# Attention and dense layers on one core: transposes alternated with products of 64 stationary columns, the activation's sums in PSUM, the last products tile by tile

## What is computed

```python
# attention: 2 batches x 8 heads, 768 rows, 64 columns; 16 clusters
q_assign = argmax(q_n . c_n); k_assign = argmax(k_n . c_n)
scores = where(q_assign == k_assign, q @ k.T / 8, -1e9)
attn = softmax(scores) @ v
# sparse layer: 1536 rows x 512, 8 experts of 1024, best expert alone
out[mask] = gate_w * eom * (relu(x[mask] @ w1[e]) @ w2[e])
# dense layers: 512 -> 2048 -> 512
h = x @ w_in
g = where(h >= 1, h, where(h <= -1, 0, (h + 1) ** 2 / 4))
return g @ w_out
```

## Time and profile before

| | us |
|---|---|
| median of three runs | 934.82 |
| lowest and highest | 929.96, 935.59 |
| the profiled execution | 934.28 |
| its span in the trace | 932.5 |
| PE busy | 826.5 (89% of the span) |
| DVE busy | 536.7 (58%) |
| ACT busy | 379.3 (41%) |
| POOL busy | 326.0 (35%) |

### The profile page before, as it was taken

The page is one execution under the profiler, slowest core; times in us unless marked ns, Lnnn a source line. Parts: engine busy times, 40 slices in busy tenths (PEclk is TensorE's granted clock), DMA queues, the critical chain, the costliest instruction groups (busy, mean ns, idle before and its releaser), DMA issues.

```text
span 932.5 us, 13746 instructions
## 1 busy us (share of the span) xinstructions
PE 826.5 (89%) x4331; PEld 682.4 (73%) x4332; DVE 536.7 (58%) x863; ACT 379.3 (41%) x762; POOL 326.0 (35%) x346
## 2 busy tenths in 40 slices
PE   4799999999999950998997997996999999999995
PEld 3688788887888840777786786784788888888884
DVE  5688788888788873334454453335645545454442
ACT  3677788777887730221211211121222322232222
POOL 4233444334432016557863863767100010010001
PEclk8899999999999985999999998999999999999998
DMA  8000223000120034889985984968000010000001
GB/s 277 26 27 26 79 88 115 25 26 25 51 98 0 1 103 159 237 279 319 332 286 172 332 281 156 332 244 271 4 1 0 1 46 1 1 23 23 1 1 45
DMA packets 46388, 105.23 MB, mean 113 GB/s; under 512 B 6544, under 2 KB 12688, under 8 KB 45328
## 3 DMA queue, kind: packets, MB, share of 16 engines
q1 hardware_dynamic: 24656, 51.48, 16.0%
q0 software_dynamic: 17408, 48.26, 15.4%
q10 hardware_dynamic: 4288, 5.03, 2.0%
HBM read 98.45 MB, written 6.32 MB: 112 GB/s over the span
## 4 chain that ended last, share of the span: by engine, by line
PE 71%; DVE 12%; issue 5%; DMA 4%; ACT 4%; POOL 2%; DVEq 1%; ACTq 0%
PE ps L1359 14%; PE ps L1346 14%; PE ps L1306 9%; PE ps L1286 9%; PE ps L1136 5%; DMA x_in<-sorted_rows 4%; DVE coef L982 3%; PE ps L1092 3%; PE ps L1122 3%; PE ps L1152 3%; PE ps L1164 2%; PE ps L1123 2%; PE ps L1150 2%; PE ps L1079 2%; POOL sorted_rows L455 1%
## 5 line engine op out<-in xcount | busy, mean ns | idle before, releaser
L344 POOL TENSOR_TENSOR weights<-staging,weights 128x2048 fp32r<-128x2048 f32 x34 | 156.5, 4616 | 32.0 <-DMA weights<-in_moe_w 24.5
L1359 PE MATMUL ps<-weights,g_t 128*128 128x512 f32 x576 | 144.6, 400 | 9.0 <-DVE g_t L1053 9.0
L1346 PE MATMUL ps<-y_t,weights 128*128 128x512 f32 x576 | 141.5, 395 | 0.0
L1359 PEld LDWEIGHTS ps<-weights,g_t 128*128 128x128 f32 x576 | 108.6, 190 | 35.6 <-DVE g_t L1053 9.9
L1346 PEld LDWEIGHTS ps<-y_t,weights 128*128 128x128 f32 x576 | 108.2, 188 | 25.7
L1306 PE MATMUL ps<-weights,h_t 128*128 x456 | 114.1, 408 | 3.9 <-issue 3.8
L1286 PE MATMUL ps<-weights,x_t 128*128 x456 | 110.9, 400 | 2.0 <-DVE x_t L976 2.0
L850 DVE TENSOR_TENSOR p_t<-ps,p_t 128x384 fp32r<-128x384 f32 x192 | 100.0, 549 | 14.8 <-ACT p_t L563 13.6
L1306 PEld LDWEIGHTS ps<-weights,h_t 128*128 128x128 f32 x456 | 87.7, 196 | 24.5 <-issue 6.0
L499 POOL DMA_INDIRECT out<-y_sb,token_u x12 | 11.9, 994 | 256.1 <-ACT y_sb L695 254.0
L1286 PEld LDWEIGHTS ps<-weights,x_t 128*128 128x128 f32 x456 | 85.4, 191 | 20.4 <-issue 2.6
(11 more groups left out here) (148 smaller groups left out, 1143.1 us busy)
## 6 DMA issues: line engine op xcount, KB each, us to landing
weights<-in_moe_w POOLq DMA_DIRECT2D x32, 1024.0 KB, 8.2
staging<-in_moe_w SPq DMA_DIRECT2D x32, 1024.0 KB, 6.1
x_in<-sorted_rows ACTq DMA_DIRECT2D x19, 258.0 KB, 4.9
weights<-in_moe_w_in POOLq DMA_DIRECT2D x4, 1024.0 KB, 8.1
staging<-in_moe_w_in SPq DMA_DIRECT2D x4, 1024.0 KB, 5.8
staging<-in_moe_w_out SPq DMA_DIRECT2D x4, 1024.0 KB, 5.7
weights<-in_moe_w_out POOLq DMA_DIRECT2D x4, 1024.0 KB, 7.1
raw<-in_q SPq DMA_DIRECT2D x16, 192.0 KB, 2.6
```

The costliest lines, as they stand in the source:

```text
L344: pool.tensor_tensor(weights[:, unit % 2, 1, c * CHUNK:(c + 1) * CHUNK], staging[:, n % 2, :], hi.bitcast(F32), ALU.subtract).then_inc(w_r ...
L1346: last = mm(ps[:, 4 + n % 2, :], wi[:, a, k, f * P:(f + 1) * P], y_ts[g % 2][:, b, k, :], start=(k == 0 and j == 0), stop=(k == KC - 1 and ...
L1359: last = mm(ps[:, t, :], g_t[:, n % 2, a, t * P:(t + 1) * P], wo[:, b, f, :], start=(f == 0 and j == 0), stop=(f == FC2 - 1 and j == 2))
```

## The change

In attention PE's list is put in another order; the instructions are the same, and so are the lists of ACT, DVE and POOL there. (1) The low products of 64 stationary columns (now `value_low`) of a step that is not the first of its half head go right behind the three transposes t=0 and t=1 of the next step, and the high ones (`value_high`) stay behind the scores. (2) In s=5 the first three cluster products alternate with the three transposes t=0, five more follow, and then the transposes t=1 alternate with the two low products. In the dense layers (3) the square goes into the PSUM bank of h, the sum is made there, and the high and low parts are read from there; the square now waits for both L1046 and L1047, and `up(n)` for the low part of n-2. (4) In the last group `up(15)` goes ahead of `down(13)`, and the last two `down` go by tiles in the order of `LAST_DOWNS`. (5) DVE copies the last tile out, where ACT did.

```diff
+LAST_DOWNS = ((14, (0, 1, 2)), (15, (0,)), (14, (3,)), (15, (1, 2, 3)))
...
             def square_and_high(n):
-                act.wait_ge(clamp_done, n + 1)
-                act.activation(g_a[:, n % 2, :], g_a[:, n % 2, :], ACT.Square, bias=half[:], scale=0.5)\
+                act.wait_ge(over_done, 2 * (n + 1))
+                act.activation(ps[:, 4 + n % 2, :], g_a[:, n % 2, :], ACT.Square, bias=half[:], scale=0.5)\
                     .then_inc(sq_done, 1)
...
-                act.activation(g_t[:, n % 2, 0, :], g_b[:, n % 2, :], ACT.Copy).then_inc(gh_done, 1)
+                act.activation(g_t[:, n % 2, 0, :], ps[:, 4 + n % 2, :], ACT.Copy).then_inc(gh_done, 1)
...
-                    dve.tensor_tensor(g_b[:, n % 2, :], g_b[:, n % 2, :], g_a[:, n % 2, :], ALU.add)\
-                        .then_inc(g_done, 1)
+                    dve.tensor_tensor(h_ps, h_ps, g_b[:, n % 2, :], ALU.add).then_inc(g_done, 1)
                     dve.wait_ge(gh_done, n + 1)
-                    dve.tensor_tensor(g_t[:, n % 2, 1, :], g_b[:, n % 2, :], g_t[:, n % 2, 0, :].bitcast(F32),
+                    dve.tensor_tensor(g_t[:, n % 2, 1, :], h_ps, g_t[:, n % 2, 0, :].bitcast(F32),
                                       ALU.subtract).then_inc(gl_done, 1)
...
+            dve.wait_ge(acc_done, NT)
+            dve.tensor_copy(y_sb[:, NT - 1, :], ps[:, GROUP - 1, :]).then_inc(last_done, 1)
...
+                    before = (h, s - 1, u) if s > 0 else None if first else (h - 1, QT - 1, un)
+                    later = before is not None and before[1] % HALF > 0
                     if s == 5 and ahead >= 2:
-                        cluster_scores(h + 2, u)
-                    transpose_probs(h, s, first)
-                    if s == 5 and ahead >= 2:
+                        for c in range(HALF):
+                            transpose_part(h, s, 0, c, first)
+                            cluster_part(h + 2, u, c)
+                        for n in range(HALF, 8):
+                            cluster_part(h + 2, u, n)
+                        for c in range(HALF):
+                            transpose_part(h, s, 1, c, first)
+                            if c < 2:
+                                value_low(h, s - 1, c, u)
                         cluster_rows(h + 2)
+                    else:
+                        for t in range(2):
+                            transpose_probs(h, s, t, first)
+                            if later:
+                                value_low(before[0], before[1], t, before[2])
...
-                    if s > 0:
-                        prob_values(h, s - 1, u, first)
-                    elif not first:
-                        prob_values(h - 1, QT - 1, un, False)
+                    if later:
+                        value_high(before[0], before[1], 0, before[2])
+                        value_high(before[0], before[1], 1, before[2])
+                    elif before is not None:
+                        values_begin(h, s - 1, u, first)
...
                 if n >= 2:
-                    pe.wait_ge(over_done, n - 1)
+                    pe.wait_ge(gl_done, n - 1)
```

More of the change, by code:

```diff
@@ L1124, in scores, with transpose_part @@
                 last.then_inc(s_done, 1)
-            def transpose_probs(h, s, first):
+            def transpose_part(h, s, t, c, first):
                 g, pair = s // HALF, s % HALF
-                if pair == 0:
-                    pe.wait_ge(exp_done, QT * h + HALF * (g + 1))
                 n = QT * h + s
-                for t in range(2):
+                if c == 0:
+                    if pair == 0 and t == 0:
+                        pe.wait_ge(exp_done, QT * h + HALF * (g + 1))
                     if not (first and s == 0):
@@ L1133, in transpose_probs @@
                         pe.wait_ge(ptl_done, 2 * n + t - 1)
-                    for c in range(HALF):
-                        k = (2 * pair + t) * P
-                        last = tr(ps[:, 4 + t, c * P:(c + 1) * P], prob[:, HALF * g + c, k:k + P], ident[:])
+                k = (2 * pair + t) * P
+                last = tr(ps[:, 4 + t, c * P:(c + 1) * P], prob[:, HALF * g + c, k:k + P], ident[:])
+                if c == HALF - 1:
                     last.then_inc(pt_done, 1)
-            def prob_values(h, s, u, first):
-                g, pair = s // HALF, s % HALF
+            def transpose_probs(h, s, t, first):
+                for c in range(HALF):
+                    transpose_part(h, s, t, c, first)
@@ new lines, in value_low, with value_high, values_begin @@
+            def value_low(h, s, t, u):
+                pe.wait_ge(ptl_done, 2 * (QT * h + s) + t + 1)
+                mm(ot_ps[0:D], v_s[:, u, 2 * (s % HALF) + t, 0:D], p_t[:, s % 2, 1, t, :], start=False, stop=False)
+            def value_high(h, s, t, u):
+                k = 2 * (s % HALF) + t
+                last = mm(ot_ps, v_s[:, u, k, :], p_t[:, s % 2, 0, t, :], start=(k == 0), stop=(k == QT - 1))
+                if t == 1:
+                    last.then_inc(pv_done, 1)
+            def values_begin(h, s, u, first):
@@ L1141, in prob_values @@
                 if s == 0:
                     pe.wait_ge(vs_done, h + 1)
-                if pair == 0 and not (first and s == 0):
-                    pe.wait_ge(norm_done, 2 * h + g)
-                for t in range(2):
-                    k = 2 * pair + t
-                    pe.wait_ge(ptl_done, 2 * (QT * h + s) + t + 1)
-                    for lo in ((0, 1), (1, 0))[t]:
-                        if lo:
-                            last = mm(ot_ps[0:D], v_s[:, u, k, 0:D], p_t[:, s % 2, 1, t, :], start=False, stop=False)
-                        else:
-                            last = mm(ot_ps, v_s[:, u, k, :], p_t[:, s % 2, 0, t, :], start=(k == 0),
-                                      stop=(k == QT - 1))
@@ L1154, in prob_values @@
-                last.then_inc(pv_done, 1)
+                if not (first and s == 0):
+                    pe.wait_ge(norm_done, 2 * h + s // HALF)
+                pe.wait_ge(ptl_done, 2 * (QT * h + s) + 1)
+                value_high(h, s, 0, u)
+                value_low(h, s, 0, u)
+                value_low(h, s, 1, u)
+                value_high(h, s, 1, u)
             def outputs_back(n, first=False):
@@ L1223, in _ @@
             attend(BH - 1, 1, False, 0)
-            prob_values(BH - 1, QT - 1, 1, False)
+            for t in range(2):
+                value_low(BH - 1, QT - 1, t, 1)
+            for t in range(2):
+                value_high(BH - 1, QT - 1, t, 1)
             outputs_back(2 * BH - 1)
@@ L1348, in up, with down @@
                 last.then_inc(f_done, 1)
-            def down(g, f):
+            def down(g, f, tiles=range(GROUP)):
                 n = g * FC2 + f
@@ L1354, in down @@
                     pe.wait_ge(w_ready, CPU * (E + 1) + f // 4 + 1)
-                for t in range(GROUP):
+                for t in tiles:
                     if f == 0 and g > 0:
@@ L1362, in down @@
                         last.then_inc(acc_done, 1)
[L1363 to L1366 removed]
+                    elif t == GROUP - 1:
+                        last.then_inc(f2_done, 1)
             pe.wait_ge(w_ready, CPU * (E + 1))
@@ L1378, in _ @@
                     down(g, f)
+            for f, tiles in LAST_DOWNS:
+                down(GROUPS - 1, f, tiles)
 R_DIFF = 2
```

48 lines of the change are left out of this document (29 added, 19 removed).

## The result

| | before | after |
|---|---|---|
| median, us | 934.81 | 940.26 |
| lowest to highest, us | 929.96 to 940.12 | 937.85 to 944.62 |
| the profiled execution, us | 934.28 | 941.56 |
| its span, us | 932.5 | 939.8 |

The ratio is 1.0058, 95% interval 1.0032 to 1.0084: slower, by about half a per cent, a small difference but clear of its interval. The forecast was 935.7 us, no measurable change, with a range of 925.5 to 944.0 over all rivals and 932.4 to 939.7 for the forecast itself.

The account below looks back on a forecast made before the run. Attention was taken as bound by a 19.57 us ring of waits over three engines, the dense layers by PE. 934.28 + 10.2 - 6.56 - 1.5 - 0.7 = 935.7 us; own range 932.4 to 939.7, wide range 925.5 to 944.

Parts of the forecast that it names:

- the clock: Start of the dense layers: PE's clock stays at 1.00 after a shorter stand, -1.5 us (0 if not).
- the end: Last dense steps and stores: last store earlier, -0.7 us (0 to -1.0).
- Part 2, the stand: Attention, step 5: PE stands 0.52 us a head at the first transpose, formerly covered by the eight cluster products.
- Part 2, the transposes: Attention, step 5: three transposes ahead of the cluster products' end, 3 x 0.054 = 0.16 us a head, plus 0.05.
- Part 1: Attention, low products behind transposes: 0.6 us of PE time saved a head, counted at nothing.
- The ring: In attention, waits over three engines, period 19.57 us; PE time saved off it counts nothing, added on it counts whole.
- PE's wait for the one-hot labels longer, not shorter: Attention, expected sign in the trace after: PE's wait for DVE's labels, about 1.05 us before, grows.
- The third rival: Attention, one-hot against POOL's split of the values: second L789 waits 1.05 us, about +1.0 a head, 949.7 us; chance 0.12.
- the deciding gap: Attention: first L789 more than 0.38 us after L380's start lets L382 in ahead of the second L789; 0.25 expected.
- Part 3: Dense layers, sums in PSUM: first sum at 0.69 to 0.75 us instead of 7.80, PE starts 6.56 us earlier.
- the longer chain: Dense layers: L1046's start to L1053's end takes 4.23 us instead of 3.63, covered in the steps between, costing nothing.
- Parts 4 and 5: Dense layers' last steps: PE stands 0.95 us ahead of step 15's tile 0, stores start 0.84 earlier; -0.7 us.

Follow-up runs that it names:

- run 6: The changed kernel with three cluster products ahead of the first transpose in s=5; 930.71 us, ratio to before 0.9954.
- Run 10: The changed kernel with the three transposes t=0 of s=5 in a row, then all eight cluster products; 934.98 us, ratio to before 1.0007.
- run 3: The kernel before with only the low values products moved behind the transposes; 935.98 us, ratio 1.0008.
- Runs 11 and 12: The kernel before, with the transposes t=0 of s=2 issued twice, 934.74 us; and with the first cluster product issued three times, 941.09 us.
- run 9: The changed kernel with three cluster products first, and ACT's copy of the first transposed probabilities ahead of the cluster scores' copy; 930.50 us, ratio to before 0.994.
- runs 7 and 8: The kernel before: sum with both inputs in SBUF, output in PSUM, 931.0 us; square in PSUM, sum with one input there, output in SBUF, 931.2 us.
- run 5: The kernel before with the dense square and sum in PSUM alone, order of last steps and last copy unchanged; 928.38 us, ratio 0.9916.

## Why the prediction was right, and where it was off

The forecast was no measurable change at 935.7 us, from a loss of 10.2 in attention and a gain of 8.8 in the dense layers. The measured 940.3 is within 1% of before and in the wide range, and both halves are there with their signs: +13.05 and -8.57. It is not right by accident, then, but one term was undersized.

It was less sure a hit than that sounds. The wide range runs from one rival to another, and so takes in results that would refute half of the account. The measured difference is clear of its interval, so it is no null, and 940.3 lies above the forecast's own range of 932.4 to 939.7, as +13.05 lies above its 12.5. That range was also added up too narrow: with the clock and the end at nothing the gain is 6.56, not 7.1, and its end 940.2. Of the 5.9 us between 935.7 and the profiled execution 2.9 are attention, 0.2 the dense layers, and 2.8 lie in the start and the sparse stage, where nothing was changed.

- **Part 2, the stand: right.** 0.52 us forecast, 0.52 measured, and run 6, which takes it away, gives back 7.4 us of attention (14 x 0.52 = 7.3).
- **Part 2, the transposes: the step that failed.** "For a transpose that is followed by 64 of them I put half, 0.054 us." They cost 0.39 a head with what was put for the wait, not 0.16 + 0.05. Three at 0.108 and 0.05 would be 0.37, the upper bound. Run 10 shows it from the other side: without the alternation the stretch is not longer. This is 0.18 x 14 = 2.5 us.
- **The rest of the period: nothing.** Over ten heads it is 0.93 longer, of which 0.51 are the stand and 0.41 the transposes. Part 1, "I count all of it at nothing", holds in the changed kernel; by itself it costs 0.1 a head (run 3).
- **The ring: right as to its effect, incomplete as to its way.** Runs 11 and 12 show it (0 off the ring, 0.36 a head on it). The prediction has the labels come out of DVE's unbroken run. DVE comes to them at about the same time, but what ends them is POOL's cast behind PE's last product with the values. And that there is a branch over ACT's exponential beside DVE's run I did not see; it has no part in this result, as both branches start at the cluster scores, but it undid my expectation of run 9.
- **"PE's wait for the one-hot labels longer, not shorter": wrong**, 1.05 in both. The wait runs from PE's own last product with the values over POOL's cast to the labels, and that way takes the same in both kernels (0.91 from the cast on).
- **The third rival** did not come, but its working was wrong. It took the 0.64 us of the two L789 as their work, where one takes 0.24 and the first is held; and by its own rows (the second L789 0.04 ahead of L382, the first 0.14 behind L380) a fixed length would make the deciding gap 0.18, not 0.38. The gap was 0.17, where I expected 0.25, and 0.24 in one head (56.86 us), without harm there: the first is held to the cast's end at any of these gaps, and the second starts about 0.05 ahead of L383 (L382 before) each time.
- **Part 3: right at the beginning.** The sum at 0.70 us, the stand 1.51 for 1.5, the chain 4.23 for 4.23, the clock at 1.00 and the twelve products 3.06 for 4.56. At the end the longer chain costs something that I had not counted, see the next point. It was only half said why: runs 7 and 8 show that the inputs count and not the output, and that the low part would have been held in the sum's place.
- **Parts 4 and 5: -0.5 instead of -0.7.** From the first `down` to the last store it takes 932.80 - 662.95 = 269.85 us now, and took 925.48 - 653.62 = 271.86, of which 1.5 was the clock's: 270.36. The wait ahead of step 15's tile 0 is 0.64, not 0.95. What I did not see is that the longer chain made them more valuable: without them run 5 needs 919.41 - 648.15 = 271.26, so they are worth 1.4, and part 3 without them loses 0.9 there (271.26 against 270.36).

By the Trainium skill (TensorE: Matmul & The Clock Gate, "LDWEIGHTS (loading the stationary operand)") a load takes a time in proportion to its stationary columns, so that 64 would need half of 128. That is what my half rested on in effect, and the runs don't bear out that a load of 64 behind a transpose makes the pair shorter: 2.04 us with the alternation, 1.99 without. These are the records of the loads in the changed kernel, 211 to 216 us, least, median and longest in ns: the transposes' (128 columns), the cluster products' (64) and the high values products' (128):

```profile
L1146 PEld LDWEIGHTS ps<-ident,prob x6: 138/138/143, 213.4 to 215.6; 128*128 128x128 f32 x6
...
L1098 PEld LDWEIGHTS ps<-qk_t,cst x8: 133/136/138, 213.6 to 214.9; 128*64 128x64 f32 x4, 80*64 80x64 f32 x4
...
L1162 PEld LDWEIGHTS ps<-p_t,v_s x2: 187/188/188, 212.1 to 212.5; 128*128 128x128 f32 x2
```

Among products the load of 64 columns is 0.05 us shorter than that of 128, but not half of it. The transposes' own load of 128 is as short as the products' load of 64. The pair shows neither difference: a transpose and the product of 384 columns behind it take 0.28 us with 64 stationary columns in the product (213.79 to 214.07), and 0.28 with 128 (from the last L1109 at 216.25 over L1132 to L1133 at 216.53).

By the Trainium skill (SBUF — State Buffer, "SBUF: two separate sides") a VectorE instruction with two inputs in SBUF and a GpSimd one that reads SBUF take a shared pair of ports as an exclusive lock: who starts first has it for the whole instruction. Runs 7 and 8 agree (7.81 and 5.85 us held, 0.69 free), and they show it to go by the inputs. So does the one-hot instruction, 0.47 us instead of 0.24, through 0.10 us after the cast. The prediction said that PE's L1107 at 212.06 contradicts this rule. That was a misreading: the first L789 does end only behind the cast, as its length shows, and the second starts 0.04 ahead of L382, so that by the rule it is not the one that has to wait.

## What to carry to other kernels

Find the ring of waits before you move anything on a busy engine: an instruction put ahead of the one that another engine waits for cost its full length in every turn, and a wait in front of it cost what the block behind it used to cover; the same kind of instruction in step 2 was free (run 11). If instructions are to be alternated with others, let as many go first as cover the first one's wait. And where GpSimd's splits held VectorE's sum for 7.8 us, one input in PSUM freed it (0.70), an output in PSUM did not (7.81); but the whole chain has to be freed, or the next instruction is held instead. Two changes in one can hide each other: the net of half a per cent here was a loss of 1.3% and a gain of 0.8%.

## What the runs showed of the hardware that was not expected

- A transpose ahead of a load of 64 stationary columns is as dear as one ahead of 128 (0.28 us with the product behind it in both): three of them in front of or between eight products of 384 columns lengthen the stretch by 0.34 to 0.39 us.
- A VectorE instruction of 128x96 elements with two inputs in SBUF takes 0.24 us alone and 0.44 to 0.47 in the two heads shown, where it starts inside a GpSimd cast of 0.51 us; it ends 0.10 us after the cast, and PE's wait of 1.05 us hangs on that.
- ScalarE takes 0.69 us to write 128x512 to PSUM (the changed kernel) and 0.72 to SBUF (the seventh), and 0.60 to copy them out of PSUM (both) where the eighth kernel takes 0.63 out of SBUF. Two instructions of the activation became 0.03 us shorter by the place of their operands.
- One PSUM input, with PSUM as the output too, costs VectorE next to nothing here: 0.70 us for the sum against 0.69.
